# Attention with decaying state ahead of a routed and a gated layer: capped scan, two early tiles over two queues, a first chunk without state products

## Chip, cores and metric

One core of a Trainium2 chip. The metric is the device time of one execution in microseconds (us); several runs are made and their median is taken.

## The reference, cut to what matters

Shapes: q, k, v and f_logit are (B=4, H=8, S=768, D=48), f32. The attention is a recurrence over time with a matrix state per head:

```
f = 1 / (1 + exp(-f_logit))
state = 0                                   # (B, H, D, D)
for t in range(S):
    state = f[:, :, t, :, None] * state + outer(k[:, :, t], v[:, :, t])
    y[:, :, t] = q[:, :, t] @ state
```

y is then laid out as 3072 tokens of 384 channels. A layer of 8 experts (one expert chosen for each token by the argmax of `x @ w_gate + modality_bias[modality_id]`) and a gated layer with RMS norm (`silu(xn @ w_gate) * (xn @ w_val) @ w_out`) follow. The change lies in the attention alone.

## The kernel before, in words

**Tiling.** Time is cut into 6 chunks of 128 steps (CH), and there are 4 batches (B), so 24 tiles; tile n is chunk n // 4, batch n % 4. Heads go in 4 pairs (PR). A tile of q, k or the logits is 128 partitions (two heads, each 48 channels at partition 0 or 64, the rest padding) by 4 x 128 columns.

**The work of a tile, by engine.** SP loads q, k and logits together (`load_qkf`, L285, two transfers, 590 KB in all) and v (`load_v`, L291). POOL clamps the logits from below (L360). ACT makes `-log f` with an exponential and a logarithm (`neg_logs`, L391 and L394). DVE makes running sums of it over time (`sums`: the scan at L455 into `sums_raw`, a multiply by `carry`, which is 0 at the first column of each head pair and 1 elsewhere, and an add) and holds them at 31 (L461, into `run`). ACT makes four exponentials of the sums (L402 `fall`, L403 `decay`, L404 `fade`, L405 `rise`). DVE scales k and q with them (L470 `kT`, L471 `qT`). PE transposes k (L561) and makes the scores (L567); ACT copies the transposed k (L413, `ks`); DVE masks the scores with a triangle (L480). PE makes the growth of the state from `ks` and v (L592, `ds_ps`), the state's share of y (L598, with start=True on the first of the four, so that it opens the accumulation), and the scores' share (L603). DVE adds the growth to the state (L488, `grown`), ACT scales that with `fade` (L420). ACT copies y (L437), PE turns it and multiplies it by the gate (L578), ACT copies the tokens (L431) and DVE sums the routing logits (L494).

**The order.** `steps` runs all engines through the same series of steps, one for each tile, four for each chunk, and each engine's part of a step is written out in its own `step`. Step n holds, on each engine in this order:

- ACT: exponentials of tile n; `neg_logs` of tile n+1; `ks` of tile n-1; state of tile n-3; tokens of tile n-3; y copy of tile n-2.
- DVE: `kT`, `qT` of tile n; sums of tile n+1; mask of tile n-1; `grown` of tile n-2; routing logits of tile n-3; then, once in four steps each, `choose` (L92 to L105, in the third step of a chunk) and `place` (L118 to L125, in the first), and in the fourth step of chunk 0 `token_bias` (L532 to L536).
- PE: transposes of tile n-1; a wait for the mask of tile n-2; scores of tile n-1; gate product of tile n-3; growth, state's share and scores' share of tile n-2; in the last step of a chunk two counting products (L109, L110).
- POOL: clamp of tile n+2; from chunk 2 on the scatter of tokens (L129).
- SP: the load of tile n waits until tile n-4 has been scaled (`scaled`), since the buffer is that tile's.

Below, T(n) is the start of the four transposes of tile n, S(n) the start of its scores, mask(n) the DVE operation on its scores.

**The start.** DVE sets the padding of tiles 0 and 1 (L274, L275), POOL the identity, the triangle, the padding of tiles 2 and 3, `state` and other constants. SP loads the logits of tile 0 first, then its q and k, then whole tiles 1, 2, 3, all on one queue. DVE clamps tile 0's logits (L540), POOL those of tile 1. PE runs 48 warm-up products (L553), each of them two passes, as soon as the triangle is made, before its first step. DVE clears `grown` (L543, 128x2048) behind the first sums.

Of the kernel before, what the change touches and what calls it, by code (L numbers as in the profile page):

```python
# [14 lines left out]
P = 128  # L15
# [29 lines left out]
LEAST_LOGIT = -40.0  # L45
WARM_UP = 48


# [85 lines left out]
def attention(nc, qkf, v, w_gate, modality, bias, ident, rt, decay, flag, x_regions):  # L134
# [9 lines left out]
    with ExitStack() as ctx:  # L144
# [18 lines left out]
        bias1 = sb("bias1", [P, NT, E])  # L163
        sums_raw = sb("sums_raw", [P, PR, P])
        exp_f = sb("exp_f", [P, PR, P])
        neg_log = sb("neg_log", [P, 2, PR, P])
        run = sb("run", [P, 2, PR, P])
        fall = sb("fall", [P, 2, PR, P])
# [10 lines left out]
        tri = sb("tri", [P, P])  # L179
        carry = sb("carry", [P, PR, P])  # L180

# [12 lines left out]
        pads_set = [sem(f"pads_set{b}") for b in range(B)]  # L194
        carry_made = sem("carry_made")
        grown_zero = sem("grown_zero")
        scanned = sem("scanned")
        f_landed = sem("f_landed")
        f_clamped = sem("f_clamped")
# [13 lines left out]
        state_done = sem("state_done")  # L213
        y_done = sem("y_done")
        yT_kept = sem("yT_kept")
        x_copied = sem("x_copied")
# [53 lines left out]
        CONSTS = 7  # L270

        def set_pads(eng, b):
# [7 lines left out]
        def _(sp):  # L280
# [17 lines left out]

            f_cols = 2 * PR * P
            sp.wait_ge(pads_set[0], 1)  # L300
            for par in range(2):
                sp.dma_start(qkf_in[par * PAD:par * PAD + D, 0, 2].rearrange("p j t -> p (j t)"),
                             qkf[0, par, :, f_cols:]).then_inc(f_landed, 16)
            sp.wait_ge(pads_set[0], 2)
            for par in range(2):
                sp.dma_start(qkf_in[par * PAD:par * PAD + D, 0, 0:2].rearrange("p a j t -> p (a j t)"),
                             qkf[0, par, :, 0:f_cols]).then_inc(qkf_landed[0], 16)
            for b in range(1, B):
                sp.wait_ge(pads_set[b], 2)
                load(0, b)  # L310
            sp.wait_ge(consts, CONSTS)
# [13 lines left out]
        def _(pool):  # L325

            nc.gpsimd.memset(ident[:], 0.0).then_inc(consts, 1)
            nc.gpsimd.memset(tri[:], 1.0).then_inc(consts, 1)
# [4 lines left out]
                                    pattern=[[1, P]], channel_multiplier=-1).then_inc(consts, 1)  # L333
            set_pads(nc.gpsimd, 2)
# [40 lines left out]

            pool.sem_inc(clamped, 1)
            clamp(0, 1)
            steps(pool, step)
# [5 lines left out]
        def _(act):  # L384
            def neg_logs(c, b, n):

                if at(c, 0) and b == 0:
                    act.wait_ge(f_clamped, 1)
# [5 lines left out]
                nc.scalar.activation(neg_log[:, b % 2], exp_f[:], ACT.Ln, bias=1.0).then_inc(log_done, 1)  # L394

            def step(c, b, half, more):
                if t := tile(c, b, 0):
                    _, s, n = t
                    act.wait_ge(run_done, n + 1)
                    wait_past(act, scaled, n - 1)  # L400
                    wait_past(act, state_done, n - 3)
                    nc.scalar.activation(fall[:, s % 2], run[:, s % 2], ACT.Exp, scale=-1.0)  # L402
                    nc.scalar.activation(decay[:, n, :], run[:, s % 2, :, P - 1], ACT.Exp, scale=-1.0)  # L403
                    nc.scalar.activation(fade[:, s], run[:, s % 2, :, P - 1], ACT.Exp, scale=-1.0).then_inc(faded, 1)  # L404
                    nc.scalar.activation(rise[:, s % 2], run[:, s % 2], ACT.Exp).then_inc(factors, 1)  # L405
                if t := tile(c, b, -1):
                    with ahead(b, 1, more):
                        neg_logs(*t)
# [30 lines left out]
            nc.scalar.preload_act_table_set("natural_log_exp_and_others")  # L439
            neg_logs(0, 0, 0)  # L440
            steps(act, step)

        @block.vector
        def _(dve):
            set_pads(nc.vector, 0)
            set_pads(nc.vector, 1)

            nc.vector.memset(carry[:], 1.0).then_inc(carry_made, 1)
            dve.wait_ge(carry_made, 1)
            nc.vector.memset(carry[:, :, 0:1], 0.0).then_inc(carry_made, 1)  # L450
# [12 lines left out]
            def step(c, b, half, more):  # L463
                if t := tile(c, b, 0):
                    _, s, n = t
                    dve.wait_ge(factors, n + 1)
                    wait_past(dve, y_done, n - 3)
                    if at(t[0], 0) and s == 0:
                        dve.wait_ge(qkf_landed[0], 32)
                    nc.vector.tensor_tensor(kT[:, s], qkf_in[:, s, 1], rise[:, s % 2], ALU.mult)  # L470
                    nc.vector.tensor_tensor(qT[:, s], qkf_in[:, s, 0], fall[:, s % 2], ALU.mult).then_inc(scaled, 1)  # L471
                if t := tile(c, b, -1):
                    with ahead(b, 1, more):
                        sums(*t)
# [74 lines left out]
        def _(pe):  # L549
            pe.wait_ge(consts, 4)  # L550

            for _ in range(WARM_UP):
                nc.tensor.matmul(ks_ps[:, 0], tri[:], tri[:], start=True, stop=True)  # L553

            def step(c, b, half, more):
                if t := tile(c, b, 1):
# [24 lines left out]
                if t := tile(c, b, 2):  # L581
# [6 lines left out]
                    pe.wait_ge(v_landed[s], (cc + 1) * 16)  # L588
                    if not at(c, CH):
                        wait_past(pe, grown_done, n)  # L590
                        for j in range(PR):
                            mm = nc.tensor.matmul(ds_ps[:, 2 * D * j:2 * D * (j + 1)], ks[:, s, j],  # L592
                                                  v_in[:, s, 2 * D * j:2 * D * (j + 1)], start=True, stop=True)
                        mm.then_inc(ds_done, 1)

                    wait_past(pe, state_done, n - 3)
# [1079 lines left out]
```

## Time and profile before

| | us |
|---|---|
| runs of the kernel before | 909.58 median of 3 (908.95 to 911.13) |
| the profiled execution's own time | 914.6 |
| its span (first to last instruction) | 912.8 |
| PE busy | 860.6 (94%) |
| DVE busy | 480.9 (53%) |
| ACT busy | 384.3 (42%) |
| POOL busy | 155.2 (17%) |
| attention: first to last product of PE | 2 to 165 |

A row of the trace gives the start in us from the span's start, the length, the engine, the line of the kernel, the operation, what is written and read, and how many of them were merged; in brackets how long the engine had sat idle and what ended that. Spans of merged products cover all of them. PEclk is TensorE's granted clock as a share of the full 2.4 GHz; 0.50 is the lower of its two levels, 1.2 GHz.

### The profile page before, as it was taken

Reading aid. Unit: us, or ns where it says so; the run is one execution under the profiler, and the core shown is the slowest. Engines: PE = TensorE matmul, PEld = TensorE weight load, DVE = VectorE, ACT = ScalarE, POOL = GpSimd, SP = SyncE. Lnnn points to the kernel's source line nnn. Section 1 sums busy time; section 2 is a strip of 40 time slices with the busy share of each in tenths; the row PEclk is TensorE's granted clock in tenths of the full one; section 3 lists DMA queues with packets and bytes.
Section 4 is the critical chain, followed back from the end, with each engine's and each line's share of the span. In section 5 each row is a group of like instructions: output and inputs, shape, how many; then the busy total and the mean of one; then the engine's idle time right before and its main releaser. Section 6 shows DMA issues by size and latency. Waiting matters only on the chain.

```text
span 912.8 us, 15598 instructions
## 1 busy us (share of the span) xinstructions
PE 860.6 (94%) x5512; PEld 786.8 (86%) x5512; DVE 480.9 (53%) x753; ACT 384.3 (42%) x737; POOL 155.2 (17%) x154
## 2 busy tenths in 40 slices
PE   7999999489989989999799999999999999999996
PEld 7888888489889989999688888888888888888885
DVE  7899998477555466566244433333334333333331
ACT  4688886246444456465232331232232133122121
POOL 5324442511117600000000020010010002001001
PEclk9899999799999999999899999999999999999999
DMA  9668761495766877784200110010020000000000
GB/s 178 130 128 172 167 147 53 165 375 206 254 211 191 254 312 253 250 262 149 87 1 1 29 42 1 1 69 0 0 69 0 0 0 34 0 0 34 0 0 34
DMA packets 33263, 97.23 MB, mean 107 GB/s; under 512 B 7920, under 2 KB 24304, under 8 KB 29776
## 3 DMA queue, kind: packets, MB, share of 16 engines
q1 hardware_dynamic: 29392, 87.38, 32.3%
q0 software_dynamic: 3840, 9.47, 2.9%
q8 instruction: 17, 0.28, 0.1%
q14 instruction: 14, 0.11, 0.0%
HBM read 76.75 MB, written 20.08 MB: 106 GB/s over the span
## 4 chain that ended last, share of the span: by engine, by line
PE 50%; POOL 0%; ACT 0%; DVE 0%; issue 0%; ACTq 0%; DVEq 0%
PE g_ps L1551 6%; PE g_ps L1552 6%; PE acc_ps L1550 6%; PE g_ps L1550 5%; PE acc_ps L1552 5%; PE acc_ps L1551 5%; PE v_ps L1552 5%; PE v_ps L1550 5%; PE v_ps L1551 5%; PE xT_ps L1545 1%; POOL out L1448 0%; ACT x_hi L1463 0%; DVE x_lo L1503 0%; DVE h_lo L1529 0%; DVE hid L1519 0%
## 5 line engine op out<-in xcount | busy, mean ns | idle before, releaser
L1516 DVE TENSOR_TENSOR gs<-g_ps,sig 128x512 f32<-128x512 f32 x72 | 49.8, 691 | 180.9 <-ACT sig L1473 180.9
L1473 ACT ACTIVATE sig<-g_ps 128x512 f32<-128x512 f32 x72 | 43.1, 598 | 176.1 <-PE g_ps L1552 176.1
L1484 ACT CAST h_hi<-hid 128x512 fp32r<-128x512 f32 x72 | 44.6, 620 | 149.6 <-DVE hid L1519 149.6
L1550 PE MATMUL acc_ps<-wo_hi,h_hi 128*128 128x384 f32 x288 | 98.5, 342 | 0.2 <-DVE h_lo L1529 0.2
L1552 PE MATMUL acc_ps<-wo_lo,h_hi 128*128 128x384 f32 x288 | 97.1, 337 | 0.0
L1551 PE MATMUL acc_ps<-wo_hi,h_lo 128*128 128x384 f32 x288 | 96.7, 336 | 0.0
L1295 DVE TENSOR_TENSOR w_lo<-w_in,w_hi 128x768 fp32r<-128x768 f32 x52 | 59.2, 1158 | 67.2 <-ACT w_hi L1186 67.0
L1326 PE MATMUL h_ps<-x_hi,w_hi 128*128 128x256 f32 x312 | 89.0, 285 | 3.0 <-DVE x_lo L1279 3.0
L1327 PE MATMUL h_ps<-x_hi,w_lo 128*128 128x256 f32 x312 | 89.0, 285 | 0.0
L1328 PE MATMUL h_ps<-x_lo,w_hi 128*128 128x256 f32 x312 | 88.9, 285 | 0.0
L1551 PE MATMUL g_ps<-x_hi,wg_lo 128*128 128x512 f32 x216 | 85.9, 398 | 0.0
L1552 PE MATMUL g_ps<-x_lo,wg_hi 128*128 128x512 f32 x216 | 85.8, 397 | 0.0
L1550 PE MATMUL g_ps<-x_hi,wg_hi 128*128 128x512 f32 x216 | 84.8, 393 | 0.9 <-DVEq L1509 0.9
L1552 PE MATMUL v_ps<-x_lo,wv_hi 128*128 128x512 f32 x216 | 84.1, 389 | 0.0
L1550 PE MATMUL v_ps<-x_hi,wv_hi 128*128 128x512 f32 x216 | 84.0, 389 | 0.0
L1551 PE MATMUL v_ps<-x_hi,wv_lo 128*128 128x512 f32 x216 | 84.0, 389 | 0.0
L1519 DVE TENSOR_TENSOR hid<-v_ps,gs 128x512 f32<-128x512 f32 x72 | 49.8, 691 | 56.8 <-PE v_ps L1552 56.8
L1326 PE MATMUL ym_ps<-w_hi,h_hi 128*128 128x384 f32 x208 | 72.1, 347 | 7.3 <-DVE w_lo L1295 7.3
L1529 DVE TENSOR_TENSOR h_lo<-hid,h_hi 128x512 fp32r<-128x512 f32 x72 | 49.8, 691 | 44.7 <-ACT h_hi L1484 44.7
L1327 PE MATMUL ym_ps<-w_hi,h_lo 128*128 128x384 f32 x208 | 70.8, 340 | 0.0
L1328 PE MATMUL ym_ps<-w_lo,h_hi 128*128 128x384 f32 x208 | 70.7, 340 | 0.0
L1326 PEld LDWEIGHTS h_ps<-x_hi,w_hi 128*128 128x128 f32 x312 | 60.4, 194 | 3.2 <-DVE x_lo L1279 3.2
(192 smaller groups left out, 1797.7 us busy)
## 6 DMA issues: line engine op xcount, KB each, us to landing
w_raw<-in_w SPq DMA_DIRECT2D x13, 1536.0 KB, 7.3
w_in<-in_w SPq DMA_DIRECT2D x13, 1536.0 KB, 7.7
qkf_in<-in_qkf SPq DMA_DIRECT2D x46, 288.0 KB, 5.2
x_regions<-zero_row SPq DMA_DIRECT2D x14, 384.0 KB, 6.7
x_group<-x_regions SPq DMA_DIRECT2D x13, 384.0 KB, 3.4
y_sorted<-x_group SPq DMA_DIRECT2D x13, 384.0 KB, 6.1
v_in<-in_v SPq DMA_DIRECT2D x24, 192.0 KB, 4.3
g_in<-in_wg SPq DMA_DIRECT2D x3, 768.0 KB, 5.7
```

Of the source, the lines that this page charges most:

```text
L1295: nc.vector.tensor_tensor(w2_lo[:, 2 * w:2 * w + 2].rearrange("p b d -> p (b d)"), w2_in[:, 2 * w * DM:(2 * w + 2) * DM], w2_hi[:, 2 * w:2 ...
L1326: nc.tensor.matmul(out, hi, rhs_hi, start=first, stop=False)
L1327: nc.tensor.matmul(out, lo, rhs_hi, start=False, stop=False)
L1328: return nc.tensor.matmul(out, hi, rhs_lo, start=False, stop=last)
L1473: nc.scalar.activation(sig[:], g_ps[:], ACT.Sigmoid).then_inc(sig_done, 1)
L1484: nc.scalar.copy(h_hi[:, fb % 2], hid[:]).then_inc(h_hi_done, 1)
L1516: nc.vector.tensor_tensor(gs[:], g_ps[:], sig[:], ALU.mult).then_inc(gs_done, 1)
L1519: nc.vector.tensor_tensor(hid[:], v_ps[:], gs[:], ALU.mult).then_inc(hid_done, 1)
L1529: nc.vector.tensor_tensor(h_lo[:, fb % 2], hid[:], h_hi[:, fb % 2].bitcast(F32), ALU.subtract).then_inc(h_split, 1)
L1550: nc.tensor.matmul(out, hi, rhs_hi, start=first, stop=False)
L1551: nc.tensor.matmul(out, lo, rhs_hi, start=False, stop=False)
L1552: return nc.tensor.matmul(out, hi, rhs_lo, start=False, stop=last)
```

## The change

The scan writes `run` itself: it adds `-log f` to the running value and takes the minimum with `cap`. `cap`, `neg_log` and `run` get a column more at the head of each pair; there `cap` and `neg_log` are 0, which brings the running value back to 0. `cap` is 31 elsewhere. The separate minimum (L461), `sums_raw` and `carry` go.

```diff
-                nc.vector.tensor_tensor_scan(sums_raw[:].rearrange("p j t -> p (j t)"),
-                                             carry[:].rearrange("p j t -> p (j t)"),
+                nc.vector.tensor_tensor_scan(run[:, b % 2].rearrange("p j t -> p (j t)"),
                                              neg_log[:, b % 2].rearrange("p j t -> p (j t)"),
-                                             0.0, ALU.mult, ALU.add).then_inc(scanned, 1)
-                dve.wait_ge(scanned, n + 1)
-
-                nc.vector.tensor_scalar(run[:, b % 2], sums_raw[:], MOST_FALL, None, ALU.min).then_inc(run_done, 1)
+                                             cap[:].rearrange("p j t -> p (j t)"),
+                                             0.0, ALU.add, ALU.min).then_inc(run_done, 1)
```

The first loads go over SP's and ACT's queues, with the logits of tiles 0 and 1 ahead of their q and k; tile 2 is split over the two queues. POOL sets the padding of tile 1 as its first work and DVE that of tile 2.

```diff
+            set_pads(nc.gpsimd, 1)                 # POOL, ahead of the identity
...
+                first_load(sp, 0, par, "f")        # SP: both halves of tile 0's logits
+            first_load(sp, 1, 0, "f")
+            for b in range(FIRST_TWO):
+                first_load(sp, b, 0, "kq")
+            second_load(sp, 0)
+            load_v(0, 0, 0)
+            sp.wait_ge(pads_set[3], 2)
+            load(0, 3)
...
             nc.scalar.preload_act_table_set("natural_log_exp_and_others")
-            neg_logs(0, 0, 0)
+            first_load(act, 1, 1, "f")             # ACT
+            for b in range(FIRST_TWO):
+                first_load(act, b, 1, "kq")
+            second_load(act, 1)
+            for b in range(FIRST_TWO):
+                neg_logs(0, b, b)
```

DVE clamps the logits of both tiles, clears `grown` and now also `yT_ps`, and only then makes the sums of tiles 0 and 1, both ahead of the first step; steps of chunk 0, batch 0 leave their sums and `neg_logs` out. POOL clears `state` after DVE's two clamps and begins its own clamps with tile 2.

```diff
-            dve.wait_ge(f_landed, 32)
-            nc.vector.tensor_scalar(qkf_in[:, 0, 2], qkf_in[:, 0, 2], LEAST_LOGIT, None, ALU.max).then_inc(f_clamped, 1)
-            dve.wait_ge(carry_made, 2)
-            sums(0, 0, 0)
+            for b in range(FIRST_TWO):
+                dve.wait_ge(f_landed[b], 32)
+                nc.vector.tensor_scalar(qkf_in[:, b, 2], qkf_in[:, b, 2], LEAST_LOGIT, None, ALU.max).then_inc(f_clamped, 1)
             nc.vector.memset(grown[:], 0.0).then_inc(grown_zero, 1)
+            nc.vector.memset(yT_ps[:], 0.0).then_inc(yT_zero, 1)
+            dve.wait_ge(cap_made, 2)
+            dve.wait_ge(tops_zero, 1)
+            for b in range(FIRST_TWO):
+                sums(0, b, b)
...
+            pool.wait_ge(f_clamped, FIRST_TWO)
+            pool.sem_inc(ordered, 1)
             nc.gpsimd.memset(state[:], 0.0).then_inc(consts, 1)
...
-            pool.sem_inc(clamped, 1)
-            clamp(0, 1)
+            pool.sem_inc(clamped, FIRST_TWO)
```

PE warms up with 22 products instead of 48. The state's share of y isn't computed for the four tiles of chunk 0, where the state is zero; the scores' products are then the first into `yT_ps`. The growth of tile 0 is made ahead of the wait for its mask.

```diff
-            for _ in range(WARM_UP):
+            for _ in range(START_WARM_UP):
...
+                    if at(c, 0) and b == 2:
+                        growth(0, 0)
                     wait_past(pe, masked, n)
...
-                    for j in range(PR):
-                        nc.tensor.matmul(yT_ps[:, j], state[:, s, j], qT[:, s, j], start=(j == 0), stop=False,
-                                         skip_group_check=True)
+                    if not at(cc, 0):
+                        for j in range(PR):
+                            nc.tensor.matmul(yT_ps[:, j], state[:, s, j], qT[:, s, j], start=(j == 0), stop=False,
+                                             skip_group_check=True)
+                    if at(cc, 0):
+                        pe.wait_ge(yT_zero, 1)
...
-                                                  scores[:, s, par, j], start=False, stop=(j == PR - 1),
+                                                  scores[:, s, par, j], start=at(cc, 0), stop=(at(cc, 0) or j == PR - 1),
```

## Rows read from the trace of the kernel before

**Rows 1.** Busy time by stretch: us, each engine (instructions), granted clock, DMA share, GB/s.

```profile
core 0: us, PE busy (x) PEld busy (x) DVE busy (x) ACT busy (x) POOL busy (x), PEclk, DMA share, GB/s
...
4.00:6.00 2.00, 2.00 (x12) 2.00 (x11) 1.90 (x4) 0.00 (x0) 2.00 (x3) 1.00 0.89 235
...
20.00:22.00 2.00, 0.79 (x6) 0.80 (x8) 1.72 (x3) 1.91 (x6) 0.00 (x0) 0.77 1.14 220
...
60.00:110.00 50.00, 47.31 (x510) 42.11 (x507) 47.59 (x99) 41.67 (x108) 21.66 (x16) 1.00 0.75 163
```

**Rows 2.** Timeline of PE at the start: start us, us, engine, line, operation.

```profile
1.96 13.57 PE L553 MATMUL ks_ps<-tri 128*128 128x128 f32 x96 [1.96 <-POOL tri L332]
15.37 0.60 PE L561 MATMUL ks_ps<-ident,kT 128*128 128x128 f32 x4
...
18.49 0.65 PE L561 MATMUL ks_ps<-ident,kT 128*128 128x128 f32 x4 [1.42 <-DVE qT L471]
21.21 2.08 PE L567 MATMUL sc_ps<-qT,kT 48*128 48x128 f32 x16 [2.07 <-DVE scores L480]
...
28.39 0.66 PE L561 MATMUL ks_ps<-ident,kT 128*128 128x128 f32 x4
```

**Rows 3.** Timeline of DVE at the start: its clamp and the clearing of `grown`.

```profile
4.71 2.00 DVE L540 TENSOR_SCALAR qkf_in<-qkf_in 128x512 f32<-128x512 f32 x1
...
10.21 1.76 DVE L543 MEMSET grown<- 128x2048 f32 x1 [0.37 <-issue]
```

**Rows 4.** Timeline of POOL: clamps of tiles 2, 4 and 19.

```profile
13.09 1.55 POOL L360 TENSOR_SCALAR qkf_in<-qkf_in 128x512 f32<-128x512 f32 x1 [1.80 <-DMA qkf_in<-in_qkf]
...
22.30 1.77 POOL L360 TENSOR_SCALAR qkf_in<-qkf_in 128x512 f32<-128x512 f32 x1 [3.54 <-DMA qkf_in<-in_qkf]
...
122.90 1.51 POOL L360 TENSOR_SCALAR qkf_in<-qkf_in 128x512 f32<-128x512 f32 x1
```

**Rows 5.** Timeline of PE: both shares of y of tile 1, and T(6).

```profile
31.93 1.08 PE L598 MATMUL yT_ps<-qT,state 128*128 128x128 f32 x8
32.94 1.08 PE L603 MATMUL yT_ps<-scores,v_in 128*48 128x128 f32 x16
...
51.91 0.66 PE L561 MATMUL ks_ps<-ident,kT 128*128 128x128 f32 x4
```

**Rows 6.** Waits from 56 to 155 us: total us, times, longest.

```profile
PE sc_ps L567 <- DVE scores L480: 5.0, 8, 1.0
```

**Rows 7.** Timeline of PE: T(17), the count, T(19), S(19), T(20), T(21).

```profile
118.48 0.66 PE L561 MATMUL ks_ps<-ident,kT 128*128 128x128 f32 x4
...
129.99 0.39 PE L109 MATMUL rt_ps<-upto,before 128*128 128x8 f32 x2
...
130.46 0.64 PE L561 MATMUL ks_ps<-ident,kT 128*128 128x128 f32 x4
132.11 1.16 PE L567 MATMUL sc_ps<-qT,kT 48*128 48x128 f32 x16 [1.02 <-DVE scores L480]
...
137.09 0.66 PE L561 MATMUL ks_ps<-ident,kT 128*128 128x128 f32 x4
...
142.65 0.66 PE L561 MATMUL ks_ps<-ident,kT 128*128 128x128 f32 x4
```

**Rows 8.** Timeline of DVE in the same stretch.

```profile
120.54 0.75 DVE L470 TENSOR_TENSOR kT<-qkf_in,rise 128x512 f32<-128x512 f32 x1 [0.31 <-ACT rise L405]
...
123.09 0.73 DVE L461 TENSOR_SCALAR run<-sums_raw 128x512 f32<-128x512 f32 x1
123.74 1.22 DVE L480 TENSOR_TENSOR scores<-sc_ps,tri 128x1024 f32<-128x1024 f32 x1
...
129.25 1.21 DVE L455 TENSOR_TENSOR_SCAN sums_raw<-carry,neg_log 128x512 f32<-128x512 f32 x1
130.49 0.43 DVE L461 TENSOR_SCALAR run<-sums_raw 128x512 f32<-128x512 f32 x1
130.84 1.22 DVE L480 TENSOR_TENSOR scores<-sc_ps,tri 128x1024 f32<-128x1024 f32 x1
```

**Rows 9.** All masks of the run: duration in ns, least, median, most.

```profile
L480 DVE TENSOR_TENSOR scores<-sc_ps,tri x24: 1209/1215/1225, 19.9 to 156.3; 128x1024 f32<-128x1024 f32 x24
```

More of the change, by code:

```diff
@@ L46 @@
 WARM_UP = 48
+START_WARM_UP = 22
+FIRST_TWO = 2
 class Routing:
@@ L163, in attention @@
         bias1 = sb("bias1", [P, NT, E])
-        sums_raw = sb("sums_raw", [P, PR, P])
         exp_f = sb("exp_f", [P, PR, P])
-        neg_log = sb("neg_log", [P, 2, PR, P])
-        run = sb("run", [P, 2, PR, P])
+        neg_log = sb("neg_log", [P, 2, PR, P + 1])
+        run = sb("run", [P, 2, PR, P + 1])
         fall = sb("fall", [P, 2, PR, P])
@@ L179, in attention @@
         tri = sb("tri", [P, P])
-        carry = sb("carry", [P, PR, P])
+        cap = sb("cap", [P, PR, P + 1])
         ks_ps = ps("ks_ps", [P, PR, P])
@@ L194, in attention @@
         pads_set = [sem(f"pads_set{b}") for b in range(B)]
-        carry_made = sem("carry_made")
+        cap_made = sem("cap_made")
+        tops_zero = sem("tops_zero")
         grown_zero = sem("grown_zero")
-        scanned = sem("scanned")
-        f_landed = sem("f_landed")
+        f_landed = [sem(f"f_landed{b}") for b in range(FIRST_TWO)]
         f_clamped = sem("f_clamped")
@@ L214, in attention @@
         y_done = sem("y_done")
+        yT_zero = sem("yT_zero")
         yT_kept = sem("yT_kept")
@@ L270, in attention, with first_load, second_load @@
         CONSTS = 7
+        def first_load(eng, b, par, part):
+            f_cols = 2 * PR * P
+            rows = slice(par * PAD, par * PAD + D)
+            if part == "f":
+                eng.wait_ge(pads_set[b], 1)
+                eng.dma_start(qkf_in[rows, b, 2].rearrange("p j t -> p (j t)"), qkf[b, par, :, f_cols:]).then_inc(f_landed[b], 16)
+            else:
+                eng.wait_ge(pads_set[b], 2)
+                eng.dma_start(qkf_in[rows, b, 0:2].rearrange("p a j t -> p (a j t)"),
+                              qkf[b, par, :, 0:f_cols]).then_inc(qkf_landed[b], 16)
+        def second_load(eng, par):
+            eng.wait_ge(pads_set[2], 2)
+            eng.dma_start(qkf_in[par * PAD:par * PAD + D, 2].rearrange("p a j t -> p (a j t)"),
+                          qkf[2, par]).then_inc(qkf_landed[2], 16)
         def set_pads(eng, b):
@@ L297, in load @@
                     load_v(*t)
-            f_cols = 2 * PR * P
-            sp.wait_ge(pads_set[0], 1)
             for par in range(2):
[L302 to L310, printed above, removed]
+                first_load(sp, 0, par, "f")
[6 more added lines that the diff above has]
+            load(0, 3)
             sp.wait_ge(consts, CONSTS)
@@ L385, in neg_logs @@
             def neg_logs(c, b, n):
-                if at(c, 0) and b == 0:
-                    act.wait_ge(f_clamped, 1)
+                if at(c, 0) and isinstance(n, int) and n < FIRST_TWO:
+                    act.wait_ge(f_clamped, n + 1)
+                    wait_past(act, log_done, n)
                 else:
@@ L393, in neg_logs @@
                 wait_past(act, run_done, n - 1)
-                nc.scalar.activation(neg_log[:, b % 2], exp_f[:], ACT.Ln, bias=1.0).then_inc(log_done, 1)
+                nc.scalar.activation(neg_log[:, b % 2, :, 1:P + 1], exp_f[:], ACT.Ln, bias=1.0).then_inc(log_done, 1)
             def step(c, b, half, more):
@@ L401, in step @@
                     wait_past(act, state_done, n - 3)
[L402 to L406, printed above, removed]
+                    nc.scalar.activation(fall[:, s % 2], run[:, s % 2, :, 1:P + 1], ACT.Exp, scale=-1.0)
+                    nc.scalar.activation(decay[:, n, :], run[:, s % 2, :, P], ACT.Exp, scale=-1.0)
+                    nc.scalar.activation(fade[:, s], run[:, s % 2, :, P], ACT.Exp, scale=-1.0).then_inc(faded, 1)
+                    nc.scalar.activation(rise[:, s % 2], run[:, s % 2, :, 1:P + 1], ACT.Exp).then_inc(factors, 1)
+                if (t := tile(c, b, -1)) and not (at(c, 0) and b == 0):
                     with ahead(b, 1, more):
@@ L445, in _ @@
             set_pads(nc.vector, 0)
[L446 to L450, printed above, removed]
+            set_pads(nc.vector, 2)
+            nc.vector.memset(neg_log[:, :, :, 0:1], 0.0).then_inc(tops_zero, 1)
+            nc.vector.memset(cap[:], MOST_FALL).then_inc(cap_made, 1)
+            dve.wait_ge(cap_made, 1)
+            nc.vector.memset(cap[:, :, 0:1], 0.0).then_inc(cap_made, 1)
             def sums(c, b, n):
@@ L467, in step @@
                     wait_past(dve, y_done, n - 3)
-                    if at(t[0], 0) and s == 0:
-                        dve.wait_ge(qkf_landed[0], 32)
+                    if at(t[0], 0) and s < FIRST_TWO:
+                        dve.wait_ge(qkf_landed[s], 32)
                     nc.vector.tensor_tensor(kT[:, s], qkf_in[:, s, 1], rise[:, s % 2], ALU.mult)
                     nc.vector.tensor_tensor(qT[:, s], qkf_in[:, s, 0], fall[:, s % 2], ALU.mult).then_inc(scaled, 1)
-                if t := tile(c, b, -1):
+                if (t := tile(c, b, -1)) and not (at(c, 0) and b == 0):
                     with ahead(b, 1, more):
@@ L550, in _, with growth @@
             pe.wait_ge(consts, 4)
-            for _ in range(WARM_UP):
+            for _ in range(START_WARM_UP):
                 nc.tensor.matmul(ks_ps[:, 0], tri[:], tri[:], start=True, stop=True)
+            def growth(s, n):
+                if isinstance(n, int) and n == 0:
+                    pe.wait_ge(v_landed[0], 16)
+                    pe.wait_ge(ks_done, 1)
+                wait_past(pe, grown_done, n)
+                for j in range(PR):
+                    mm = nc.tensor.matmul(ds_ps[:, 2 * D * j:2 * D * (j + 1)], ks[:, s, j],
+                                          v_in[:, s, 2 * D * j:2 * D * (j + 1)], start=True, stop=True)
+                mm.then_inc(ds_done, 1)
             def step(c, b, half, more):
@@ L588, in step @@
                     pe.wait_ge(v_landed[s], (cc + 1) * 16)
-                    if not at(c, CH):
-                        wait_past(pe, grown_done, n)
+                    if not at(c, CH) and not (at(c, 0) and b == 2):
+                        growth(s, n)
+                    wait_past(pe, state_done, n - 3)
+                    if not at(cc, 0):
                         for j in range(PR):
[L592 to L596, printed above, removed]
-                    for j in range(PR):
-                        nc.tensor.matmul(yT_ps[:, j], state[:, s, j], qT[:, s, j], start=(j == 0), stop=False,
-                                         skip_group_check=True)
+                            nc.tensor.matmul(yT_ps[:, j], state[:, s, j], qT[:, s, j], start=(j == 0), stop=False,
+                                             skip_group_check=True)
+                    if at(cc, 0):
+                        pe.wait_ge(yT_zero, 1)
                     for j in range(PR):
```

1 line of the change is left out of this document (removed).

## Prediction

> **What bounds the kernel now.** Only the attention is touched, so I read it alone: first the busy time by stretch, then PE's timeline, then the waits, then DVE's timeline where PE waits. What follows the attention starts from its end and should move with it as a whole.
>
> In the middle PE and DVE are both nearly full: from 60 to 110 us PE was busy 47.31 of 50 us, DVE 47.59, ACT 41.67 [rows 1]. They take turns. From T(20) to T(21) PE went through a step without a wait: 5.56 us; the count adds 130.46 - 129.99 = 0.47 once in four steps. That floor is 4 x 5.56 + 0.47 = 22.7 us for a chunk, and T(17) to T(21) took 24.17 [rows 7]. The difference is PE's wait for the mask: 5.0 us from 56 to 155 us [rows 6] and as starts, which include what the transposes would have covered, 5.5. One large wait comes per chunk, behind `choose`: S(19) came 1.65 us after T(19), where the transposes alone need 0.6 [rows 7].
>
> At the start three things are to be seen. The transfers are full (share 0.89 at 4 us, 1.14 at 20 us) and POOL's clamps wait for them: tile 2 at 13.09, tile 4 at 22.30 [rows 1, 4]. PE's 48 warm-up products hold T(0) until 15.37, long after `qT` of tile 0. And the clock fell to 1.2 GHz near 21 us, after a stretch in which PE had done little but T(1): the step from S(1) to T(2) took 28.39 - 21.21 = 7.18 us [rows 1, 2]. The same products at full clock take 4.98 (S(19) to T(20)) less the gate product, about 1.0, so 4.0 [rows 7].
>
> **The minimum goes.** It costs 0.35 us of DVE where nothing disturbs it (130.49 to 130.84) and 0.65 where POOL's clamp runs (123.09 to 123.74, clamp at 122.90) [rows 4, 8]. I follow one chunk from T(17), at 0. `kT` of tile 18 is released by ACT at 2.06 (120.54 - 118.48). mask(18) started 10.30 later (130.84 - 120.54), and two minima lie between, 0.65 + 0.35: 9.30 is left. PE starts 1.27 after a mask starts (132.11 - 130.84). So S(19) comes at 2.06 + 9.30 + 1.27 = 12.63, and 4.98 + 5.56 later the next T(21): 23.17 against 24.17 [rows 7, 8]. PE without any wait would have S(19) at 11.6 + 0.6 = 12.2, so a wait of 0.43 stays. The other steps' waits (0.1 to 0.5) go: there the mask ends 0.3 us or more before PE wants it. Four such waits of 0.43 stay of some 5.6: **3.9 us** saved.
>
> The unknown is where the disturbance by the clamp goes. The lower bound: it moves on to what stands in the minimum's place and 0.30 stays, 4 x 0.30 less, 2.7 us. The mask stands there, and all 24 masks took 1.209 to 1.225 us, though clamps ran beside some [rows 9]. I take it as gone. The Trainium skill ("SBUF — State Buffer", Who interferes with whom) says the same from the ports: a VectorE operation with at most one input in SBUF does not contend with GpSimd, and the mask reads PSUM and the triangle. By that rule the sum is 3.9, by a lock that catches any successor 2.7.
>
> The scan has 516 elements for 512, 1%: nothing. Whether add and minimum run as fast as multiply and add no row shows: at best as now (1.21 [rows 8]; I see no way to less, as the elements follow one another), at worst twice that. I take it as equal, since kind, type and length are the same.
>
> **The start.** Bytes ahead of tile 2's landing are the same as before (logits and q, k of two tiles, then tile 2), and so for tiles 3 and 4. The transfers are full, so a second queue brings at most the ramp, some tenths. I keep 13.1 and 22.3 for the clamps and take nothing for the queues; ACT issues its four transfers while it would wait anyway (it did nothing from 4 to 6 us [rows 1]).
>
> DVE's first clamp took 2.00 [rows 3] beside POOL's clearing of `state`; now that waits, and the clamp should take the minimum's 0.43 [rows 8]. But the gain, 1.5 us, is spent: the clearing of `grown`, 1.76 [rows 3], and of `yT_ps` (bounds 0.4 and 1.2, a 512-column operation as the minimum or as the scan; I take 0.6) now stand ahead of the first scan, which so starts near 8.5, about as before. Two scans end near 11.0, `kT` and `qT` of tile 0 at 12.4. PE: triangle about 1.1 us later, as POOL first sets pads; 44 warm-up passes from 3.1, at the slow pace of 6 per us [rows 1] until 10.4, at mixed pace until 9.5. So T(0) near 12.4 instead of 15.37.
>
> Then the landings rule. Clamp of tile 2 until 14.6, exponential and logarithm 1.3 (two of ACT's some eleven operations of a tile, 5.0 us in all: 41.67 / 50 x 24.17 / 4 [rows 1, 7]), scan 1.25, mask(0) 1.2: **S(1) at 18.5 instead of 21.21**. The growth of tile 0 lies before it. From here two cases.
>
> *Clock falls (my forecast).* Before S(1) PE does T(0), S(0), T(1), one growth: some 3 us of work in the 9 from 9.5 on, as thin as what stood before the fall at 21 [rows 1, 2]. The next two steps run at half clock: S(1) 2.0, scores' share 1.5, T(2) at 22.0, S(2) 22.9, T(3) at 29.2 with the clock back on the way (28.39 before was T(2)). T(4) comes 0.6 + 4.0 later, 33.8 (no state's share: 32.94 - 31.93 = 1.01 less [rows 5]). There ACT, with 5.0 us a tile, and `token_bias` on DVE hold the masks back: S(4) about 35.0, T(5) 39.0, S(5) 40.1, T(6) at 45.0. Before it was 51.91 [rows 5]: **6.9 us**.
>
> *Clock holds.* T(3) at 26.3, S(3) 28 (scan of tile 4 first, which waits for the landing at 22.30), T(4) 32, S(4) 34.0, T(6) at 43.65: 8.3 us. Only 1.4 more, since the landing of tile 4 and ACT take the rest. The four state's shares, 4.0 us, are in these sums; alone they would be the most that they could bring.
>
> **Sum.** 6.9 + 3.9 = 10.8 us. On the profiled execution: 914.6 - 10.8 = 903.8. Its time stands 5.0 over the median; the sum carries over to 909.6 - 10.8 = **898.8**.
>
> **Rivals.**
> 1. Clock holds: 8.3 + 3.9 = 12.2, 897.4. For it: the denser chunk 0. Against: the gaps before 18.5. 0.22.
> 2. Long slow spell: PE stays at 1.2 GHz until T(4), then 37.8 against 39.55, T(5) 42.4 against 46.3: 3.9 at the start, 7.8 in all, 901.8. For it: less warm-up and less work. Against: before, the clock came back in one dense step. 0.15.
> 3. The early part does not do what it says: T(6) is set by landings and ACT, nothing is gained before it, and only the 3.9 stays, 905.7. Against: tile 6's clamp had landed by 30 us. 0.05.
> 4. Slower than before: the scan with a minimum in its feedback takes longer, at worst twice. Place: DVE, which is nearly full [rows 1]. Then a chunk is 24.17 - 1.4 + 4 x 1.21 = 27.6, 3.4 more, about 17 over five chunks, less 7 to 8 of the start: 919. It decides from about 0.7 us more per scan (5 x (4 x 0.7 - 1.4) = 7). Against: both forms feed one result back for each element. The Trainium skill ("DVE: opcode table, instruction layouts, handler registers and perf-mode slots", 6. Datapath and trigger behaviour) lays the scan's half throughput to how far the result is routed back, which would make the two equal; no row shows it. 0.05.
>
> The forecast has 0.48; 0.05 is left for what I don't see, half of it within 0.3% or above. The later stages keep their own slow-clock spells, which may fall elsewhere and move the time by 1 to 2 us.
>
> **Range.** The forecast's own: 2.7 for 3.9 gives 900.0, late clock spells 1.7 either way. Cases 1 and 2 belong inside: 897.4 - 1.7 and 901.8 + 1.7, so 895.7 to 903.5. Outside are cases 3, 4 and tails, under 0.2. A measurement of this kernel can tell about 0.3%, 2.7 us: faster means below 906.9. Faster 0.92, same 0.03, slower 0.05.
>
> **What would show it.** The scan's row: 1.2 us, no operation behind it, masks still 1.22. T(6) near 45; S(1) near 18.5; the clamp of tile 4 still at 22.3. PE's wait for masks from T(7) on at about 0.4 once a chunk, T to T 23.2 there. First scan near 8.5 and DVE clamps of 0.43. Clock 0.5 somewhere from 18 to 28, or, for case 1, nowhere; for case 2 beyond 31. I am wrong if the scan exceeds 1.5 us, if masks lengthen, if tile 4 lands later than 23, or if the attention ends earlier and the end of the kernel does not.

## The result, and the profile after

The kernel after took 900.63 us (median of 4 runs, 897.40 to 901.93), beside 909.27 for the kernel before (908.74 to 911.13): a ratio of 0.9895, 95% interval 0.987 to 0.992. Run again later on another chip, it stood at 0.985 of before (0.982 to 0.988). The forecast was 898.8, range 895.7 to 903.5. One run of before, beside the first experiments, took 1713.63 us, nearly double, and no ratio here uses it.

The profiled execution after took 900.71 us, with a span of 899.0 against 912.8. In the attention the difference is plain. PE's timeline of after, the start first (start us, length, engine, line, operation, count):

```profile
3.32 7.52 PE L579 MATMUL ks_ps<-tri 128*128 128x128 f32 x44 [3.32 <-POOL tri L350]
...
13.86 0.66 PE L597 MATMUL ks_ps<-ident,kT 128*128 128x128 f32 x4 [3.02 <-DVE qT L493]
...
17.10 1.09 PE L597 MATMUL ks_ps<-ident,kT 128*128 128x128 f32 x4 [1.12 <-ACT ks L432]
...
17.98 1.86 PE L587 MATMUL ds_ps<-v_in,ks 128*128 128x96 f32 x8
...
19.77 2.08 PE L605 MATMUL sc_ps<-qT,kT 48*128 48x128 f32 x16
...
23.66 1.12 PE L597 MATMUL ks_ps<-ident,kT 128*128 128x128 f32 x4
...
33.85 0.66 PE L597 MATMUL ks_ps<-ident,kT 128*128 128x128 f32 x4
...
36.08 1.16 PE L605 MATMUL sc_ps<-qT,kT 48*128 48x128 f32 x16 [1.57 <-DVE scores L502]
...
45.70 0.66 PE L597 MATMUL ks_ps<-ident,kT 128*128 128x128 f32 x4
...
143.30 0.63 PE L597 MATMUL ks_ps<-ident,kT 128*128 128x128 f32 x4
```

T(0) is at 13.86 (15.37 before), S(1) at 19.77 (21.21), T(2) at 23.66 (28.39), T(6) at 45.70 (51.91) [rows 2, 5], and T(23) at 143.30 (154.53). So T(6) is 6.2 us earlier, and 5.0 more are won between T(6) and T(23), which took 97.6 us instead of 102.6. Busy time by stretch of after (the columns of [rows 1]):

```profile
14.00:16.00 2.00, 1.98 (x20) 1.51 (x19) 1.42 (x2) 0.78 (x2) 1.16 (x1) 0.77 1.24 163
18.00:20.00 2.00, 2.00 (x11) 1.83 (x12) 1.70 (x3) 1.97 (x6) 1.03 (x1) 0.50 1.05 187
24.00:26.00 2.00, 2.00 (x20) 1.62 (x18) 0.36 (x1) 2.00 (x6) 0.08 (x1) 0.67 1.05 193
50.00:100.00 50.00, 49.93 (x540) 44.44 (x539) 45.60 (x93) 43.77 (x115) 25.29 (x17) 1.00 0.80 172
```

The clock fell to 1.2 GHz early again, here during S(0), and came back between 24 and 26 us. In the middle PE is now busy 49.93 of 50 us, and it is DVE that waits. The waits of after, from 52 to 144 us (total, times, longest), the answer to [rows 6]:

```profile
DVE kT L492 <- ACT rise L424: 5.0, 10, 0.7
...
PE sc_ps L605 <- DVE scores L502: 0.5, 1, 0.5
```

PE waited once for a mask, 0.5 us. All scans and all masks of after (ns: least, median, most):

```profile
L480 DVE TENSOR_TENSOR_SCAN run<-neg_log,cap x24: 1169/1230/1637, 9.8 to 134.9; 128x516 f32<-128x516 f32 x24
```

```profile
L502 DVE TENSOR_TENSOR scores<-sc_ps,tri x24: 1191/1197/1225, 17.7 to 145.1; 128x1024 f32<-128x1024 f32 x24
```

The scan with add and minimum costs what the one with multiply and add cost (median 1.23 us for 516 elements, 1.21 in [rows 8] for 512).

The first work of DVE in after:

```profile
4.73 0.42 DVE L563 TENSOR_SCALAR qkf_in<-qkf_in 128x512 f32<-128x512 f32 x1
...
6.70 0.43 DVE L563 TENSOR_SCALAR qkf_in<-qkf_in 128x512 f32<-128x512 f32 x1 [1.54 <-DMA qkf_in<-in_qkf]
...
7.50 1.76 DVE L564 MEMSET grown<- 128x2048 f32 x1 [0.38 <-issue]
...
9.37 0.48 DVE L565 MEMSET yT_ps<- 128x512 f32 x1
...
9.76 2.34 DVE L480 TENSOR_TENSOR_SCAN run<-neg_log,cap 128x516 f32<-128x516 f32 x2
```

The clamp of tile 0 fell from 2.00 us [rows 3] to 0.42, but tile 1's logits came only at 6.70 and the first scan at 9.76, later than before. POOL's clamps of tiles 2 and 4 stand where they stood [rows 4]:

```profile
13.40 1.76 POOL L379 TENSOR_SCALAR qkf_in<-qkf_in 128x512 f32<-128x512 f32 x1 [2.38 <-DMA qkf_in<-in_qkf]
...
21.82 1.49 POOL L379 TENSOR_SCALAR qkf_in<-qkf_in 128x512 f32<-128x512 f32 x1 [2.79 <-DMA qkf_in<-in_qkf]
```

### The profile page after: what moved, and what is told of

It is laid out like the page before. It is cut to its first block, busy times and chain, and to the rows that moved or that the text cites. A ratio compares the mean times of both kernels' runs of the same rounds, so it can differ in the third digit from the quotient of the medians.

```text
span 899.0 us, 15413 instructions
## 1 busy us (share of the span) xinstructions
PE 852.4 (95%) x5428; PEld 778.4 (87%) x5428; DVE 468.5 (52%) x732; ACT 384.9 (43%) x737; POOL 158.6 (18%) x153
## 4 chain that ended last, share of the span: by engine, by line
PE 51%; POOL 0%; ACT 0%; DVE 0%; issue 0%; ACTq 0%; DVEq 0%
PE g_ps L1588 6%; PE g_ps L1589 6%; PE acc_ps L1587 6%; PE g_ps L1587 6%; PE acc_ps L1589 6%; PE acc_ps L1588 6%; PE v_ps L1587 5%; PE v_ps L1589 5%; PE v_ps L1588 5%; PE xT_ps L1582 1%; POOL out L1485 0%; ACT x_hi L1500 0%; DVE x_lo L1540 0%; DVE hid L1556 0%; DVE h_lo L1566 0%
```

## The experiments

In the table, times are of the profiled execution of each, in us; "T(7) to T(23)" is the steady part; the ratio is to before in the same rounds, with its interval.

| kernel | S(1) | T(6) | T(7) to T(23) | T(23) | median | ratio |
|---|---|---|---|---|---|---|
| before | 21.21 | 51.91 | 96.5 | 154.53 | 909.27 | |
| after | 19.77 | 45.70 | 91.6 | 143.30 | 900.63 | 0.9895 (0.987 to 0.992) |
| e1, old scan in after | 20.23 | 49.88 | 96.1 | 151.96 | 907.33 | 0.9952 (0.9935 to 0.997) |
| e2, new scan in before | 19.42 | 48.98 | 92.0 | 146.99 | 902.56 | 0.990 (0.988 to 0.992) |
| e3, state's shares kept | 19.34 | 48.24 | 91.8 | 146.09 | 899.02 | 0.986 (0.983 to 0.989) |
| e4, 48 warm-up products | 19.18 | 44.58 | 91.6 | 142.16 | 897.99 | 0.984 (0.982 to 0.987) |
| e5, one queue | 19.44 | 47.01 | 92.4 | 145.45 | 898.57 | 0.985 (0.983 to 0.988) |
| e6, 34 warm-up products | 17.56 | 42.74 | 91.6 | 140.33 | 898.51 | 0.986 (0.983 to 0.989) |
| e8, clearing later | 20.01 | 47.17 | 91.6 | 144.77 | 899.93 | 0.986 (0.983 to 0.989) |
| e9, 34 products, bias earlier | 18.32 | 43.08 | 91.6 | 140.67 | 897.40 | 0.984 (0.981 to 0.987) |
| e10, one queue, 34 products | 17.89 | 42.05 | 91.2 | 139.23 | 909.12 | 0.985 (0.983 to 0.987) |
| e13, e6 again | 17.49 | 41.84 | 91.6 | 139.42 | 904.82 | 0.981 (0.979 to 0.984) |
| e11, after again | 19.63 | 45.58 | 91.2 | 142.78 | 908.32 | 0.985 (0.982 to 0.988) |
| e12, before again | 20.92 | 51.32 | 96.5 | 153.94 | 922.57 | 1.000 (0.997 to 1.002) |

The first two rows ran together; then e1, e2, e4, e6, beside a before of 911.96; then e3, e5, e8, e9, beside 911.44; then the last four, beside 921.69, on a chip on which both kernels took longer (before by 13.3 us, after by 7.7). Medians are compared inside such a group only; where the kernel after itself is missing from a group, only ratios can be set beside each other.

### e1: the old scan in after

```diff
-                nc.vector.tensor_tensor_scan(run[...], neg_log[...], cap[...], 0.0, ALU.add, ALU.min).then_inc(run_done, 1)
+                nc.vector.tensor_tensor_scan(sums_raw[...], cap[...], neg_log[...], 0.0, ALU.mult, ALU.add).then_inc(scanned, 1)
+                dve.wait_ge(scanned, n + 1)
+                nc.vector.tensor_scalar(run[:, b % 2], sums_raw[:], MOST_FALL, None, ALU.min).then_inc(run_done, 1)
```

(Shortened. `cap` holds 1 instead of 31 here, `sums_raw` is back, and the sums of tile 1 wait for those of tile 0.)

> The kernel after with the scan undone alone (multiply and add into a buffer, then a minimum of its own). T(n) is the start of the transposes of tile n. Theory (two separate gains: the scan's, tile after tile, about 5 us, and the start's, about 6): T(6) stays near 46, at most 1 us later than after's 45.7; from T(7) to T(23) PE waits for masks again and the stretch takes 96 us as before, not 91.6; in all about 905.5 us. Rival (the start does it all, and the waits for masks went because the start shifted who is ahead): the stretch stays near 92 us and the time near 900.6.

The steady part took 96.1 us, as the theory said; the median was 907.33, where about 905.5 was expected. T(6) was 4.2 us later than after's, where at most 1 was expected. Waits from 56 to 153 us of e1, and two rows of its PE timeline from S(4) on:

```profile
PE sc_ps L611 <- DVE scores L508: 4.6, 8, 1.0
```

```profile
37.11 1.42 PE L611 MATMUL sc_ps<-qT,kT 48*128 48x128 f32 x16 [2.08 <-DVE scores L508]
...
38.45 2.03 PE L622 MATMUL x_ps<-turn_gate,yT 128*128 128x104 f32 x8
```

PE's waits are back. Before S(4) it waited 2.08 us, and then the clock was at 1.2 GHz once more for a while (the gate product took 2.03 us instead of 1.14), which after's profile does not have. Up to T(4) e1 was only 0.5 us behind after (34.37 against 33.85); the other 3.7 us were lost with the spell. e5 and e8 had such a second spell near 37 us too, though they have the new scan. So most of what e1's T(6) lost is a spell that comes in some executions, and T(6) is not as good a landmark as the steady part.

### e2: the new scan alone

The edit of the change's first diff, on the kernel before.

> The kernel before with the new scan alone. Theory: T(6) within 1 us of before's 51.9, T(7) to T(23) in 91.6 to 92.5 us instead of 96.5, in all about 904.5 us. My prediction's step (a wait of 0.43 us stays once a chunk): T(7) to T(23) in 92.6 to 93.3, about 905.4. Rival (start does it all): 909.

92.0 us from T(7) to T(23): the scan gives 4.5 of the 4.9 us of the steady part without the rest of the change. The remaining wait that I had forecast once a chunk is there twice, at S(15) and S(19), 0.9 us in all. Together 7.5 us at T(23), a ratio of 0.990, which is no worse than the 0.9895 of the whole change in its first runs: by the medians alone the rest of the change would not be seen. The median, 902.56, lay 1.9 us below the theory's. The scan also moved T(6), by 2.9 us, of which the theory allowed 1. S(1) already came 1.8 us earlier, behind an earlier mask; I take that for the missing minima, since DVE stands in the chain from a tile's logits to the mask there too, but the start differs between two executions of before as well (T(6) at 51.91 and 51.32).

### e4, e6, e13: more warm-up

```diff
-START_WARM_UP = 22
+START_WARM_UP = 48        # e4; 34 in e6 and e13
```

> The kernel after with 48 warm-up products instead of 22. They end near 16.4 us, so T(0) comes at 16.4 instead of 13.9. Theory (what limits the start is the landing of tiles 2 and 4 and the clock): the clock stays at its upper level through chunk 0, S(1) still comes near 19.5, T(6) between 44 and 45.7, time equal to after or up to 1.5 us less. Rival (the early T(0) is what the shorter warm-up brings): T(6) at 47.5 or later and 902.5 us or more.

> The kernel after with 34 warm-up products instead of 22: they end near 13.4, just before T(0) at 13.9. Theory (the half clock from 14 to 24 us costs about 1.4 us, as the prediction's two cases differ): no half clock before 30 us, T(3) near 27, T(6) near 44.3, time about 899.2. Rival (landing of tiles and ACT set T(6) whatever the clock): clock up, T(6) still 45.4 or later, time 900.6.

> The kernel after with 34 warm-up products once more, beside after itself on the same chip. Theory (the half clock in chunk 0 is worth some 2 to 3 us of T(6)): 1 to 3 us below after in the same rounds, no half clock before 30 us, T(6) 42.5 to 43.5. Rival (the gain is the spread of slow-clock spells later in the kernel): within 0.7 us of after.

e6's timeline of PE, and the clamp of tile 2 in e6:

```profile
3.33 10.22 PE L579 MATMUL ks_ps<-tri 128*128 128x128 f32 x68 [3.33 <-POOL tri L350]
...
14.10 0.66 PE L597 MATMUL ks_ps<-ident,kT 128*128 128x128 f32 x4 [0.55 <-DVE qT L493]
...
15.78 0.66 PE L597 MATMUL ks_ps<-ident,kT 128*128 128x128 f32 x4
16.27 1.03 PE L587 MATMUL ds_ps<-v_in,ks 128*128 128x96 f32 x8
17.56 1.16 PE L605 MATMUL sc_ps<-qT,kT 48*128 48x128 f32 x16 [0.26 <-DVE scores L502]
```

```profile
12.27 1.51 POOL L379 TENSOR_SCALAR qkf_in<-qkf_in 128x512 f32<-128x512 f32 x1 [1.37 <-DMA qkf_in<-in_qkf]
```

Here PE sat idle 0.55 us before T(0), not 3.02, and everything up to T(6) ran at 2.4 GHz. T(1) took 0.66 us instead of 1.09, the growth 1.03 instead of 1.86, S(1) came 2.2 us earlier and T(6) 3.0 (3.7 in e13 against e11). That is double what the theory gave the clock, 1.4 us.

Not all of it is the clock, however. In both profiles tile 2 was also ready earlier: its clamp began at 12.27 in e6 and 12.12 in e13, beside 13.40 in after and 13.32 in after again, and ended 1.4 us earlier in both pairs. This landing varies with 22 products too (12.39 in e8, 12.85 in e3). Counted from the end of that clamp, S(1) came 3.8 to 3.9 us later in the four profiles with 34 products and 4.6 in after, after again and e3; T(6) came 27.9 to 29.0 us later with 34 products and 30.5 to 30.6 in after and after again. By this count, an estimate, 1.6 to 2.6 us of T(6) are the clock's and the rest the landing's. The early landing may however bring nothing while the clock is down: e8, whose clearing stands elsewhere, had it and reached T(4) at 33.68, beside 33.85 in after. So the clock's share lies between 1.6 and 3.7 us, and these runs do not separate it further.

In the same rounds e13 stood at 0.981 and after at 0.985: the medians differ by 3.5 us, but the intervals overlap. And e10, also with 34 products and in the same rounds, took 909.12, 0.8 us more than after again, although its T(23) came 3.6 us earlier. The profiles show the gain in the attention; on the whole time it is not shown. With 48 products T(0) was late (16.10), S(1) was not (19.18), and T(6) came at 44.58, with a spell at half clock near 34 us. The rivals of e4 and e6 fall: with the clock up T(6) does move. That of e13, which is about the time, is not ruled out.

### e3: the state's shares kept

```diff
-                    if not at(cc, 0):
+                    if True:
...
-                                                  scores[:, s, par, j], start=at(cc, 0), stop=(at(cc, 0) or j == PR - 1),
+                                                  scores[:, s, par, j], start=False, stop=(j == PR - 1),
```

> The kernel after with the state's share of y computed in chunk 0 as well (on a state of zeros). Theory (PE is the one that is late between S(1) and T(3), at half clock, so the share of tile 0 costs 1.9 us there and that of tile 1 about 1.0; those of tiles 2 and 3 partly vanish in waits): T(6) 2 to 3.5 us later than after's 45.7, and the time as much. Rival (landings and ACT's chain set T(6), the shares lie in PE's waits): T(6) within 0.7 us of 45.7, time within 1 us.

T(6) came at 48.24, 2.5 us later, as the theory said. e3's timeline shows the share of tile 0 on the path at half clock:

```profile
21.35 2.07 PE L633 MATMUL yT_ps<-qT,state 128*128 128x128 f32 x8
23.35 1.95 PE L640 MATMUL yT_ps<-scores,v_in 128*48 128x128 f32 x16
```

Its median does not show that loss: 0.986, beside after's 0.9895 and 0.985 in other groups, and 0.985 and 0.986 for e5 and e8 in its own. Single runs spread over 4.4 us in e3. So by the trace the shares are worth 2.5 us, and on the whole time that is not shown.

### e5, e10: one queue

All first loads from SP, in the same order (`first_load(sp, b, par, ...)` in loops over b and par, then `second_load(sp, par)`), those of ACT taken out; e10 also has 34 warm-up products.

> The kernel after with all first loads on SP's queue, in the same order. Theory (the transfers are full from 4 us on, a second queue brings only tenths at the ramp): clamp of tile 1 and of tile 2 within 0.6 us of after's 6.70 and 13.40, T(6) within 0.7 us of 45.7, same time. Rival (two queues bring the landings forward): clamp of tile 2 at 14.4 or later, T(6) 1 us or more later.

> The kernel after with all first loads on SP's queue and 34 warm-up products. With one queue the logits of tile 1 were clamped at 5.07 us instead of 6.70 and T(0) came at 12.23. Theory (landing of tiles 2 to 4 and the clock set the start): PE is busy until about 13.2 and the clock stays up, S(1) near 17.5 to 18, T(6) 42.5 to 43.5, the same as with 34 products and two queues. Rival (the earlier first sums carry through): T(6) at 41.8 or earlier. As a version it should be at or below 0.986 of before.

Two rows of DVE in e5, its second clamp and its first scans:

```profile
5.07 0.42 DVE L561 TENSOR_SCALAR qkf_in<-qkf_in 128x512 f32<-128x512 f32 x1
...
8.13 2.34 DVE L478 TENSOR_TENSOR_SCAN run<-neg_log,cap 128x516 f32<-128x516 f32 x2
```

One queue brings tile 1's logits 1.6 us earlier; the theory allowed 0.6 us. The half that came late with two queues is not the one on ACT, issued at 1.33 us and landed 2.5 us later. It is SP's third transfer, issued near 2.4 us: it took 4.3 us to land, and the same transfer 2.2 in e5. In after, ACT issued its q and k from 2.54 on, close behind it; in e5 no q or k was issued before 3.30. That the transfers of q and k slowed it fits these times, but no run isolates it. It is worth nothing in the end: the clamp of tile 2 came at 13.32 against 13.40, S(4) at 35.79 against 36.08, and T(6) of e10 at 42.05 against e13's 41.84 (both a little earlier than the 42.5 to 43.5 expected). e5's own T(6), 47.01, lies outside the expected 0.7 us, behind a second spell at half clock near 37 us. So no gain from the second queue is seen.

### e8: the clearing behind the sums

```diff
-            nc.vector.memset(grown[:], 0.0).then_inc(grown_zero, 1)
-            nc.vector.memset(yT_ps[:], 0.0).then_inc(yT_zero, 1)
...
             for b in range(FIRST_TWO):
                 sums(0, b, b)
+            nc.vector.memset(grown[:], 0.0).then_inc(grown_zero, 1)
+            nc.vector.memset(yT_ps[:], 0.0).then_inc(yT_zero, 1)
```

> The kernel after with the clearing of grown and of yT_ps behind the two first sums instead of ahead of them. Theory (T(0) is early enough, the landing of tile 2 limits S(1)): first scan near 7.3 instead of 9.76, but the clearing then stands ahead of kT of tile 0, so T(0) at 13.3 to 13.9, S(1) and T(6) within 0.7 us, same time. Rival (the sums of tile 0 are on the path): T(6) and the time 1 to 2 us less.

```profile
7.21 1.23 DVE L480 TENSOR_TENSOR_SCAN run<-neg_log,cap 128x516 f32<-128x516 f32 x1
```

The first scan came 2.5 us earlier, S(1) at 20.01 and S(4) at 35.95, where after has 19.77 and 36.08: no gain, as the theory said. T(6) came at 47.17, again behind a half-clock spell near 37 us.

### e9: the routing bias one step earlier

```diff
-                if at(c, 0) and b == B - 1:
+                if at(c, 0) and b == B - 2:
                     token_bias()
```

> 34 warm-up products and the routing bias made one step earlier on DVE, where it waits for ACT's exponentials of tile 3. Theory (after the clock, what holds S(4) back 1.6 us is the mask of tile 3 behind that bias, 1.5 us): S(4) - T(4) falls from about 1.9 to under 1.0, T(6) 1 to 1.5 us earlier than with 34 products alone, time about 1 us less. Rival (ACT's chain from the landing of tile 4 holds the mask as much): T(6) within 0.4 us of that kernel's.

T(3) and S(3) in e9's timeline of PE and, behind them, T(4) and S(4):

```profile
26.25 0.66 PE L597 MATMUL ks_ps<-ident,kT 128*128 128x128 f32 x4
...
28.05 1.16 PE L605 MATMUL sc_ps<-qT,kT 48*128 48x128 f32 x16 [1.14 <-DVE scores L502]
...
32.10 0.66 PE L597 MATMUL ks_ps<-ident,kT 128*128 128x128 f32 x4
...
32.69 1.16 PE L605 MATMUL sc_ps<-qT,kT 48*128 48x128 f32 x16
```

S(4) followed T(4) after 0.59 us, as forecast (2.27 in e6), but the wait had moved one tile forward: 1.14 us before S(3), behind a DVE that had made the bias just ahead of `kT` of tile 3. T(6) was at 43.08 against 42.74, after an S(1) that already came 0.8 us later (18.32 against 17.56), ahead of anything that the edit touches. The rival's number held, though not for its reason: the work was not hidden in the new place either.

### e11, e12: both kernels again

> The kernel after once more, to see how far its time stands from before's on another chip and whether the landmarks repeat. Theory: T(6) 45 to 47.5, T(6) to T(23) 97.6 to 98.5, ratio to before 0.985 to 0.989; what it loses against the 11 us of the attention lies in half-clock spells of later stages that differ from execution to execution. Rival (the later stages give some of it back in a fixed way): from the start of the expert stage to the end 2 us or more longer than in before's profile.

> The kernel before once more with a profile. Theory: landmarks repeat (T(6) 51 to 52.5, T(6) to T(23) 102 to 103), while the stretch from the start of the expert stage to the end differs by 1 to 4 us from the first profile's 742.3 us, with the sum of the half-clock spells. Rival: the start itself varies by several us from execution to execution, so that T(6) lies outside 50.5 to 53.5.

These landmarks repeat within 0.6 us: T(6) at 45.58 and 51.32, T(23) at 142.78 and 153.94. So does the attention's gain, 11.2 us at T(23) in both pairs. The rest, from the start of the expert stage (POOL's `ones_e`, at 170.54 us in before) to the end of the span, took 742.3 us in before and 750.9 in before again, 739.7 in after and 748.7 in after again: 9 us more on this chip with either kernel, where 1 to 4 were expected, and no longer after than before, so that the rival of e11 falls. Busy time from 300 to 400 us, before again and after again:

```profile
300.00:400.00 100.00, 92.00 (x623) 90.47 (x624) 54.44 (x62) 51.14 (x72) 8.82 (x9) 0.93 0.71 240
```

```profile
300.00:400.00 100.00, 99.02 (x679) 98.10 (x679) 59.46 (x66) 55.09 (x78) 0.94 (x2) 0.97 0.76 249
```

Half-clock spells of the later stages differ between executions in place and length (a clock of 0.93 here, 0.98 in before's first profile). Over the profiles taken on the first chips this rest ranged from 737.1 to 743.9 us, whatever the kernel. In that spread 2 us at the start vanish. On the last chip it was 748.0 (e13) to 753.0 us (e10), which is why e10's earlier T(23) does not show in its time. Why that chip needs more stays open.

## Why the prediction was right, and where it was off

**Sum and side.** 10.8 us were forecast; the profiles show 11.2 at T(23), the medians 8.6 with this chip and 13.4 on another. The time, 900.63, lies inside the range, 1.8 above the forecast. That the time came so near is partly luck, as the medians of one and the same pair of kernels differ by 8.6 us on one chip and 13.4 on the other; the sum is better judged by T(23). The two halves were also right in order: 6.9 and 3.9 forecast for the start and the steady part, 6.2 and 5.0 found.

**The steady part.** The term that was mis-sized is the wait of 0.43 us that was to stay once in a chunk. It stayed once in all, at S(19); from T(17) to T(21), the chunk with that wait, after took 23.25 us, and 23.17 were forecast. The others had none. By taking only the two minima out of before's 10.30 us I had taken over the rest as it stood there, with a `qT` of 1.13 us that began 0.01 us behind POOL's clamp (128.18), where it takes 0.68 with no clamp beside it:

```profile
128.19 1.13 DVE L471 TENSOR_TENSOR qT<-qkf_in,fall 128x512 f32<-128x512 f32 x1
```

But the clamp moves when the load is issued at another time. The answer lies in DVE's and POOL's timelines of after, in the same step of two chunks:

```profile
95.52 1.22 DVE L480 TENSOR_TENSOR_SCAN run<-neg_log,cap 128x516 f32<-128x516 f32 x1
96.66 1.20 DVE L502 TENSOR_TENSOR scores<-sc_ps,tri 128x1024 f32<-128x1024 f32 x1
...
118.35 1.64 DVE L480 TENSOR_TENSOR_SCAN run<-neg_log,cap 128x516 f32<-128x516 f32 x1
119.91 1.19 DVE L502 TENSOR_TENSOR scores<-sc_ps,tri 128x1024 f32<-128x1024 f32 x1
```

```profile
95.55 2.48 POOL L379 TENSOR_SCALAR qkf_in<-qkf_in 128x512 f32<-128x512 f32 x1 [1.13 <-DMA qkf_in<-in_qkf]
...
118.10 1.68 POOL L379 TENSOR_SCALAR qkf_in<-qkf_in 128x512 f32<-128x512 f32 x1 [0.84 <-DMA qkf_in<-in_qkf]
```

At 95.5 the scan was first by 0.03 us: it took 1.22 and the clamp 2.48 instead of 1.5. At 118.1 the clamp was first by 0.25: it took 1.68 and the scan 1.64, and that is the one wait of 0.5 us. POOL's loss costs nothing. In these two places the one that started first kept its time, or nearly. Four more scans of after took 1.64 us though the clamp began 0.45 to 0.62 us behind them (at 60.62, 83.40, 106.24 and 129.41); there a scatter of tokens (L131) was already running on POOL when the scan began, so POOL was first there too. PE did not wait behind those four, nor behind the long scan at 49.34. Of after's long scans only that at 118.35, in the step behind `choose`, made PE wait.

The other profiles bear this out. Of the three scans just ahead of S(11), S(15) and S(19), a long one, and with it the wait, comes in none in e10 and after again, in one in after and e13, in two in e2 and in all three in e5, and T(7) to T(23) takes 91.2, 91.6, 92.0 and 92.4 us: 0.4 us each. My 3.9 us had the wait at all three and at S(7), where none of these six profiles has it. Which case comes is set by some tenths in the start of a clamp, and no term of my sum had that.

The Trainium skill ("SBUF — State Buffer", Who interferes with whom) calls the shared ports an exclusive lock, and says of VectorE's 2-port modes that whoever issues first has them for the whole instruction while the other is fully blocked; of an operation with two inputs in SBUF, as the scan, it says that it contends with a GpSimd instruction that reads SBUF. The trace comes near a full block where the scan was first (the clamp took 1.0 us longer, and a full block would make 1.2); where the clamp was first the scan lost only 0.4 of the 1.4 us that this would make. The masks, with one input in SBUF, never exceeded 1.225 us, as taken. A further tenth in each tile came from the mask starting 1.14 us after the scan, where the minimum had started 1.24 after it [rows 8].

**The start.** Right: the clamps of tiles 2 and 4 begin near where they did (13.40 and 21.82, forecast 13.1 and 22.3), the second queue gives nothing that is seen (e5, e10), the earlier clamp is spent (e8), the state's shares are worth less than their 4 us (2.5 in e3), the clock falls. T(6) was forecast at 45.0 and came at 45.70. Off, in parts that partly cancel: S(1) came at 19.77 instead of 18.5. I had T(1) right behind S(0), but its transposes wait until ACT has copied tile 0's, and ACT does that only behind `neg_logs` of tile 2: T(1) came at 17.10, and it and the growth ran at half clock before S(1). What made up for it is the clock's return: from T(2) to T(3) I had 7.2 us and it took 5.4, so that T(3) and T(4) came at 29.04 and 33.85 (forecast 29.2 and 33.8), though T(2) had been 1.7 us late. That T(4) was met is therefore luck. The 0.7 us at T(6) arose behind it, in a wait at S(4) that I had 1.0 us too short. The half clock itself I priced at 1.4 us, as the difference of my two cases; it costs 1.6 us at least and 3.7 at most (e6, e13). The first scan came at 9.76, not 8.5, because tile 1's logits landed late on two queues, without effect on T(6).

**The rivals.** "Clock holds" did not happen in after; more warm-up makes it happen (e6, e13). The long slow spell until T(4) did not come, and shorter second spells did in e1, e5 and e8. The slow scan is ruled out by its row, and "the early part does nothing" by T(6), 6.2 us earlier (2.9 of them come with the new scan alone in e2).

## What to carry to other kernels

Where two engines take turns and both are nearly full, take work off the one that the other waits for, and read the gain from where the wait stood: the minimum, 0.35 to 0.65 us in each tile, was worth 4.5 us of the steady part by itself (e2), and all the rest of the change 0.4 at most. When a start is shortened, fill what becomes idle in front of TensorE: 22 warm-up products left 3 us of idle time and the clock fell; 34 kept it up in four profiles of four, and the attention ended 2.6 to 3.6 us earlier, part of which may be an earlier landing. Whether the whole time gains is not shown: versions with 34 stood at 0.981 to 0.986 of before and the change as it was made at 0.985 and 0.9895, with intervals that overlap. And judge a gain of 2 us at the start by landmarks in the trace, of more than one execution and with the landings beside them, not by medians of runs that spread over 2 to 10 us.

## What was unexpected of the hardware

Moving half of the first transfers to a second queue made the data of tile 1 later, not earlier (clamp at 6.70 against 5.07 us), while tile 2 landed at the same time (13.40 against 13.32). And a scan slowed by POOL's clamp lost 0.41 us whether it began 0.2 us into the clamp (e13, 45.47) or 0.5 (after again, 33.15), while a clamp slowed by a scan lost up to 1.0 (after, 95.55): before these runs I had taken the price as one number.
